# A third buffer for decayed queries, another order of the first loads, and tail sums read first

## What is computed

```python
def _attn_ref(q, k, v):
    scores = scale * np.matmul(q, k.transpose(0, 1, 3, 2))
    gamma = 1.0 - 2.0 ** (-5.0 - np.arange(H, dtype=np.float32))
    Dmat = np.where(rel >= 0, gamma[:, None, None] ** rel[None, :, :], 0.0)
    return np.matmul(scores * Dmat[None], v)

def _moe_ref(x, w_gate, w_val, w_out, rms_g):
    rms = np.sqrt(np.mean(x * x, axis=-1, keepdims=True) + 1e-06)
    xn = x / rms * rms_g
    g = xn @ w_gate
    return (g / (1.0 + np.exp(-g)) * (xn @ w_val)) @ w_out
```

## Time and profile before

| | us |
|---|---|
| median of 3 runs | 807.5 |
| lowest and highest | 806.5, 807.71 |
| profiled execution | 807.88 |
| its span | 805.6 |
| TensorE busy | 786.5 (98%) |
| VectorE busy | 463.6 (58%) |
| ScalarE busy | 433.1 (54%) |
| GpSimd busy | 423.1 (53%) |

### The profile page before, as it was taken

One profiled execution on the slowest core, in us unless ns is written; L12 is line 12 of the kernel. 1 busy time (PEld: TensorE's weight loads), 2 busy tenths in 40 slices (PEclk: granted clock), 3 DMA queues, 4 the chain that ended last, 5 costly groups with the idle time before them and its releaser, 6 DMA issues.

```text
span 805.6 us, 15080 instructions
## 1 busy us (share of the span) xinstructions
PE 786.5 (98%) x5103; PEld 699.6 (87%) x5103; DVE 463.6 (58%) x809; ACT 433.1 (54%) x846; POOL 423.1 (53%) x422
## 2 busy tenths in 40 slices
PE   8998999999999999999999999999999999999996
PEld 7887898996889999688999977798888888888885
DVE  3489675675556767643666637574545545555451
ACT  3566655564666556466655534454544545545452
POOL 2579986786767878667678625640122112211111
PEclk9999999999999999999999999999999999999999
DMA  9984251213411242221114212244446455564552
GB/s 320 325 279 158 100 189 53 74 58 108 129 53 53 75 136 79 92 66 53 43 63 138 73 52 70 82 161 152 150 154 195 151 168 159 162 199 147 172 166 92
DMA packets 48029, 103.66 MB, mean 129 GB/s; under 512 B 6624, under 2 KB 8035, under 8 KB 47494
## 3 DMA queue, kind: packets, MB, share of 16 engines
q1 hardware_dynamic: 43702, 92.09, 35.6%
q0 software_dynamic: 3840, 10.23, 4.2%
q10 hardware_dynamic: 432, 0.63, 0.2%
HBM read 93.49 MB, written 11.80 MB: 131 GB/s over the span
## 4 chain that ended last, share of the span: by engine, by line
PE 87%; POOL 6%; issue 2%; DMA 1%; DVE 1%; ACT 1%; SPq 0%; POOLq 0%; DVEq 0%; ACTq 0%
PE banks L1743 10%; PE banks L1745 9%; PE banks L1744 9%; PE banks L1805 6%; PE banks L1806 6%; PE banks L1807 6%; PE banks L1998 6%; PE banks L1996 6%; PE banks L1997 6%; PE banks L1727 5%; PE banks L1729 5%; PE banks L1728 5%; POOL AL L594 2%; PE banks L1842 2%; PE banks L1672 1%
## 5 line engine op out<-in xcount | busy, mean ns | idle before, releaser
L1743 PE MATMUL banks<-BH,AH 128*128 128x384 f32 x504 | 170.4, 338 | 2.5 <-ACT p_m L1377 1.5
L1745 PE MATMUL banks<-BH,AL 128*128 128x384 f32 x504 | 168.8, 335 | 0.0
L1744 PE MATMUL banks<-BL,AH 128*128 128x384 f32 x504 | 168.7, 335 | 0.0
L1743 PEld LDWEIGHTS banks<-BH,AH 128*128 128x128 f32 x504 | 94.6, 188 | 8.9 <-issue 5.0
L594 POOL TENSOR_TENSOR AL<-s_ab,AH 128x1024 fp32r<-128x1024 f32 x36 | 88.4, 2454 | 24.5 <-ACT AH L1331 24.5
L749 POOL DMA_INDIRECT out<-yo,rec_cur x24 | 22.9, 955 | 147.5 <-ACT yo L1579 145.0
L1744 PEld LDWEIGHTS banks<-BL,AH 128*128 128x128 f32 x504 | 94.7, 188 | 0.1
L1745 PEld LDWEIGHTS banks<-BH,AL 128*128 128x128 f32 x504 | 94.6, 188 | 0.0
L1805 PE MATMUL banks<-dH,hidH 128*128 128x512 f32 x216 | 85.7, 397 | 1.6 <-DVE hv L937 0.9
L608 POOL TENSOR_TENSOR dL<-wraw,dH 128x256 fp32r<-128x256 f32 x72 | 61.5, 873 | 47.8 <-ACT dH L1347 47.6
L1807 PE MATMUL banks<-dH,hidL 128*128 128x512 f32 x216 | 84.4, 391 | 0.0
(11 more groups left out here) (208 smaller groups left out, 1669.6 us busy)
## 6 DMA issues: line engine op xcount, KB each, us to landing
wraw<-w_moe SPq DMA_DIRECT2D x168, 256.0 KB, 3.1
wraw<-w_moe SPq DMA_DIRECT2D x36, 512.0 KB, 3.6
vr<-v_rows SPq DMA_DIRECT2D x15, 320.0 KB, 4.6
qt<-q_t SPq DMA_DIRECT2D x16, 288.0 KB, 5.1
kt<-k_t SPq DMA_DIRECT2D x15, 288.0 KB, 4.2
kr<-k_rows SPq DMA_DIRECT2D x16, 256.0 KB, 3.5
hid<-w_out_t SPq DMA_DIRECT2D x3, 1024.0 KB, 7.7
y_rows<-y_sb SPq DMA_DIRECT2D x4, 768.0 KB, 6.6
```

Source lines behind the costliest of these rows:

```text
L1743: mm(to, wh, bh, start=first and k == 0, stop=False, skip_group_check=True)
L1744: mm(to, wh, bl, start=False, stop=False, skip_group_check=True)
L1745: i = mm(to, wl, bh, start=False, stop=k == 1, skip_group_check=True)
```

## The change

It does five things. (1) SP issues k and q of unit 1 ahead of its rows of k and v. (2) WARM is 7, not 10. (3) `qd` has three buffers, which lie in the memory of BL's last two parts, and GpSimd makes the decayed query of unit u+2 in turn u, before `add_squares(u-1)`; in turn u it waits for that load and, as before, for `s_attn` to reach u. (4) `mean_square` is split: at u = 5 and 9 ScalarE takes the tail right behind `evacuate`, ahead of `decay_k`, at u = 14 even ahead of `evacuate(13)`; the full columns stay where they were. (5) `from_state` reads the buffer (u+2) % 3.

```diff
 QK = 3
+QD = 3
...
-WARM = 10
+WARM = 7
...
         BH = sb("BH", [P, 7, 2, HALF], F32R)
+        q_stack = ExitStack()
+        sb_in(q_stack, "ahead", [P, 5, 2, HALF])
+        qd = sb_in(q_stack, "qd", [P, QD, SEQ - CHUNK])
+        q_stack.close()
         BL = sb("BL", [P, 7, 2, HALF], F32R)
...
-        qd = sb("qd", [P, 2, SEQ - CHUNK])
...
             for u in range(1, UNITS):
-                load_kv(u)
-                load_qk(u)
+                if u == 1:
+                    load_qk(u)
+                    load_kv(u)
+                else:
+                    load_kv(u)
+                    load_qk(u)
...
-                p, i3, hp = u % 2, u % QK, u % PAIRS
+                p, i3, hp = (u + 2) % QD, u % QK, u % PAIRS
                 pool.wait_ge(s_inqk[i3], (u // QK + 1) * N_QK)
-                wait(pool, s_attn, u - 1)
+                wait(pool, s_attn, u - QD + 1)
...
             pool.wait_ge(s_decay[1], 16)
+            spread_decay(1)
+            decay_q(1)
             for u in range(UNITS):
-                if u + 1 < PAIRS:
-                    spread_decay(u + 1)
-                if u + 1 < UNITS:
-                    decay_q(u + 1)
+                if u + 2 < PAIRS:
+                    spread_decay(u + 2)
+                if u + 2 < UNITS:
+                    decay_q(u + 2)
                 if u > 0 and (u - 1) % PAIRS > 0:
                     add_squares(u - 1)
...
-            def mean_square(b):
+            def mean_square(b, tail):
...
-                for cols, sums in norm_columns(b):
-                    S.activation(r[:, cols], sums, ACT.Abs_reciprocal_sqrt, scale=1.0 / DM, bias=eps[:, 0:1])
-                    i = S.activation(m[:, cols], sums, ACT.Identity, scale=1.0 / DM, bias=eps[:, 0:1])
-                    i.then_inc(s_mstail if cols == TCOLS else s_ms, 1)
+                cols, sums = norm_columns(b)[0 if tail else 1]
+                S.activation(r[:, cols], sums, ACT.Abs_reciprocal_sqrt, scale=1.0 / DM, bias=eps[:, 0:1])
+                i = S.activation(m[:, cols], sums, ACT.Identity, scale=1.0 / DM, bias=eps[:, 0:1])
+                i.then_inc(s_mstail if tail else s_ms, 1)
...
             for u in range(UNITS):
+                if u == 14:
+                    mean_square(2, True)
                 if u > 0:
                     evacuate(u - 1)
+                if u in (5, 9):
+                    mean_square((u - 5) // PAIRS, True)
                 if u + 2 < UNITS:
                     decay_k(u + 2)
                 if u in (5, 9, 14):
-                    mean_square((u - 5) // PAIRS)
+                    mean_square((u - 5) // PAIRS, False)
```

More of the change, by code:

```diff
@@ L1513, in _ @@
             high_b(0, NT4)
-            mean_square(BATCH - 1)
+            mean_square(BATCH - 1, True)
+            mean_square(BATCH - 1, False)
             copy_m5(0)
@@ L1671, in from_state @@
                         to = banks[r, o, c * CHUNK:(c + 1) * CHUNK] if c < FULL else banks[r, o + 1, OUT_T]
-                        mm(to, state[r, p, c - 1:FULL * HD:FULL], qd[r, p, (c - 1) * CHUNK:(c - 1) * CHUNK + w],
+                        mm(to, state[r, p, c - 1:FULL * HD:FULL], qd[r, (u + 2) % QD, (c - 1) * CHUNK:(c - 1) * CHUNK + w],
                            start=c in (1, FULL), stop=False, skip_group_check=True)
```

## The result

The changed kernel takes 809.97 us in the median of 22 executions (806.8 to 815.0); the kernel before takes 807.54 beside it. The ratio is 1.0031, interval 1.0019 to 1.0043: 0.3% slower, where 806.0 was forecast. The profiled execution took 811.48 us with a span of 809.2, against 807.88 and 805.6 before. Lines of code move: scores are L1664 (L1649 before), sums L1652 (L1637), from_state L1687 (L1672), the norms L1710 and L1711 (L1695, L1696), the query L556 and L559 (L548, L551), the sum of squares L572 (L564).

What follows compares the result with a forecast made beforehand. TensorE, busy 786.5 of 805.6 us, was taken as the bound. Gains of 0.05 us up to unit 10, 1.2 in the late turns and 0.25 behind the attention made 1.5: 807.5 to 806.0 us, range 803.6 to 808.4.

Steps and rivals of the forecast that it cites:

- What bounds the kernel, and which stalls go: TensorE bounds the kernel; the change aims at its attention-phase stalls, 6.5 us in all, between 0 and 83 us.
- the seven: TensorE stalls: 2.0 and 0.4 us for DMA, 0.79, 0.33 and 1.09 for ScalarE, 1.14 and 0.74 for GpSimd.
- Entry: Scores of unit 1 at 8.7; 1.4 us gained at full clock (taken) or 0.3 at half; unit 3's scores 0.85 sooner.
- Seven products of ones, nought "apart from the clock": At the start: TensorE free 1.3 us sooner, but unit 0's v rows hold the first products; gain nought.
- The norms wait behind a query that waits for its load: norm(0) and norm(1) each wait 1.0 to 1.4 us for GpSimd's sum; norm(0) starts at 32.0 to 32.4.
- Its size at norm(1): At norm(1), the wait for GpSimd's sum loses 1.2 us (1.0 to 1.5).
- What the wait costs: Half clock priced at the entry, 1.1 us more; no clock term behind the norm waits.
- sums wait for slow transfers: Rival: units 6 and 10 land 1.6 us later, both norms too, 3.2 us more: 809.2 us; chance 0.12.
- Late turns, 1.2 us: After unit 10: query waits go, norm(2) waits for VectorE's state near 74.3; 1.2 us gained (0.7 to 1.35).
- The rival in which VectorE holds the late turns: Stalls for GpSimd become waits for VectorE, only 0.4 us of the late gain left: 807.1 us; chance 0.12.
- Tails: ScalarE's earlier tails remove 0.79 and 0.33 us at u=5 and 9; the third's 1.09 taken as 1.0.
- Behind the attention: TensorE's waits for p_m and g: VectorE's s_ab runs without GpSimd beside it; 0.25 us gained (0 to 0.45).

Runs made afterwards that it cites:

- b3: The kernel before with only the loads of unit 1 turned round (q and k ahead of the rows): ratio 0.9988, median 806.30 us.
- b5: The kernel before with only seven products of ones instead of ten: ratio 1.0012, median 808.07 us.
- a1: The changed kernel with GpSimd's sum of squares ahead of the decayed query in every turn: ratio 1.0001, median 808.05 us.
- a4: The changed kernel with 5 and 14 unused products of ones in the waits before norm(0) and norm(1): ratio 1.0008, median 808.10 us.
- b1: a1 with ScalarE's high_S(1) moved behind the tail of the third mean square: ratio 1.0026, median 808.72 us.
- c4: The changed kernel with k and q of every unit loaded ahead of its rows, not only unit 1's: ratio 0.9979, median 806.12 us.
- a3: The kernel before with only the third buffer and the query of unit u+2 made in turn u: ratio 1.0022, median 809.72 us.
- b4: The kernel before with only the mean-square tails read ahead: ratio 0.9989, median 806.55 us.
- c2: The changed kernel with ten products of ones again: ratio 1.0044, median 811.7 us.
- d0: c4 run once more, unchanged: ratio 0.9988, median 806.76 us.
- d1: c4 with two query buffers, the query made one unit ahead: ratio 0.9992, median 806.53 us.
- a2: The changed kernel without its third buffer, the query of unit u+1 made in turn u again: ratio 0.9978, median 806.12 us.
- c1: The kernel before with only unit 1's loads turned round and the tails read ahead: ratio 0.9983, median 806.36 us.
- c3: The changed kernel with ten products of ones and the sum ahead of the query in turns 4 and 8 only: ratio 0.9996, median 807.51 us.
- d2: c4 with the sum of squares ahead of the query in turn 12: ratio 0.9999, median 807.29 us.

## Why the prediction was wrong

- *What bounds the kernel, and which stalls go*: right. Six of the seven went in after, and of the first 0.21 us is left.
- *Entry*: the place was right. Scores of unit 1 start at 9.14 (forecast 8.7) and run at 1.2 GHz, the end that was kept and not taken; scores of unit 3 at 19.23, later than forecast (18.85), and the 0.39 before unit 5 is gone. In b3, with ten products, it came at the full clock, and norm(0) 1.3 us sooner than before.
- *Seven products of ones, nought "apart from the clock"*: wrong. They cost 1.0 us in b5, and its lower clock is the likely reason. It isn't the whole story, since in profiled executions with seven products the clock stayed up four times (a1, a4, b1, c4) and with ten it fell four times (before, a3, b4, c2), and the ten of c2 brought after nothing. The Trainium skill, "TensorE: Matmul & The Clock Gate", Part 1, has the gate follow how busy TensorE has lately been, and the same kernel come out differently from run to run; both agree with what is seen here, the second by the executions of c2 (807.4 us at 0.998, 815.2 at 0.989).
- *The norms wait behind a query that waits for its load*: right mechanism, named with its instructions. norm(0) agreed to 0.1 us.
- *Its size at norm(1)*: this is the step that failed. 1.2 us (1.0 to 1.5) was forecast, 3.1 came. The working's own terms (the sum ends at 5.0 us of the turn, the norm could start at 4.07) give 0.9. It took one landing of 5.0 us from one row and GpSimd's times where nothing ran beside it. The terms measured: landing 1.2 us more, the query 0.6 more (1.09 and 0.83, for which 1.00 and 0.32 would have stood alone), the sum 0.2 more. The landing of q of unit 10 was 5.0 to 6.7 us over the kernels that load the rows first, so the row of before was the lowest of them (4.6 to 5.2 in the four that load q first).
- *What the wait costs*: the second failure. The half clock was priced at the entry but not behind the norm waits. A wait of 1.9 us (a3) left the clock alone, one of 3.1 brought it down for 6.8 us and cost 2.45 more, a term that the sum had at nothing.
- *The rival "sums wait for slow transfers"* (809.2, chance 0.12) was the case, for norm(1) alone and with the clock in the place of the second norm; that its total came so near is in part luck. It had the right row for it (7.9 us), and its chance was too low: two landings stood against each other and the argument went by one.
- *Late turns, 1.2 us*: 0.4 in after, 0.5 by the stretch (d0 against d1). That norm(2) would be released by VectorE's state, with 0.4 us to win there, was right in kind and near in size (0.3); the time was 80.02 in after and not 74.3. But the working took the stalls behind it as removable too, and VectorE has no room before it. The third buffer turns waits for the query into waits for VectorE (0.87 and 1.81 in after, 1.69 in c4). The rival in which VectorE holds the late turns, with 0.4 left, named this size and this engine.
- *Tails*: 0.9 us by b4, forecast 0.8 + 0.3 for the first two. Right; of the third's 1.0 nothing with two buffers, as it turns into 1.04 for the query.
- *Behind the attention*: right in kind and too small, 0.56 us (0.89 to 0.33) against 0.25 (0 to 0.45). With the late turns it makes 1.0 of a forecast 1.45.

The sum as it was measured in the profiled executions, up to the first product of the next stage (+4.1 us): entry and DMA stall -0.9 up to norm(0)'s wait, norm(0) +1.0, both norms' tails -1.1, norm(1) +3.1, clock +2.45, late turns -0.4. Against the forecast, the clock (2.45), norm(1) (1.9), the late turns (0.8) and the entry (0.3) make up the difference.

The fastest versions are c4, a2 and c1 (0.9978 to 0.9983, c4 0.9988 when it ran again as d0), which can't be told apart: edits 1 and 4 with the query in two buffers, or all of the change with every q loaded first.

## What to carry to other kernels

Work made ahead in an in-order queue is only free if its input is there: before moving an instruction earlier, ask what it waits for, who stands behind it, and load that input earlier first. A landing time taken from one row can be the lower end of a range, as here, and a wait on TensorE of three microseconds should be priced with the clock that follows it. Where two engines are full, removed stalls come back; the stretch between two fixed points over several kernels shows that better than the list of stalls. And the releaser that a profile names for a wait for several semaphores has to be held against the end times of all of them: here that changed the engine.

## What the runs showed of the hardware

- TensorE's granted clock fell to 1.2 GHz in a wait of 3.1 us and stayed there for 6.8 us, over instructions without a gap. From norm(0) on, waits of 1.0 to 1.9 us left it at 2.4 GHz; at or behind 2.35 (c3), 3.06 (a1), 3.53 (c2) and 3.88 us (b1) it fell too, at 2.76 (d2) it didn't. In the first 16 us it fell behind shorter ones (1.77 us in after).
- The column of the granted clock says 1.00 in the first microseconds of every trace, but the products of ones take 0.23 us a record there (20 in 4.61 us, before) and 0.12 in a4's wait (27 in 3.18 us). So the column may not tell the clock of the start.
- Ordinary products of ones in the wait keep it up (a4), though nobody needs them.
- One and the same load of 288 KB, unit 10's q, took between 4.6 (d0) and 6.7 us (c2) from issue to landing; unit 3's took 7.9 in the kernel before.
- GpSimd's query of 64 columns took 0.32 us alone and 0.83 beside VectorE's normalisation (it ends at 51.54, that one at 51.36), and VectorE's s_ab 0.42 alone and 1.61 beside the sum of squares (53.36 and 53.08). Each ends 0.2 to 0.3 us behind the other engine's. The second half of that normalisation took 1.55 us beside the query, and 0.81 in the kernel before. The Trainium skill, "SBUF — State Buffer", "SBUF: two separate sides", has one engine hold the shared port pair for a whole instruction while the other blocks; the trace agrees.
